# First MLP of a fused attention and MLP kernel: first eight units taken one by one, powers in another order

## The reference

```python
q_pool = q.reshape(B, H, S // 2, 2, D).mean(axis=3)
attn = softmax(q_pool @ k^T / sqrt(D));  x = attn @ v        # 2 x 8 heads
# first MLP, d_ff 2048
h = x @ w_in;  h2 = h * h;  h3 = h2 * h
P = a[0] + a[1] * h + a[2] * h2 + a[3] * h3
Q = 1.0 + np.abs(b[0]) * np.abs(h) + np.abs(b[1]) * h2
x = (P / (Q + 1e-06)) @ w_out
# second MLP, d_ff 1536
rms = sqrt(mean(x * x) + 1e-06);  xn = x / rms * rms_g
out = (silu(xn @ w_gate) * (xn @ w_val)) @ w_out2
```

## Time and profile before

| | us |
|---|---|
| median of 3 runs | 706.7 (705.28 to 706.94) |
| the profiled execution | 705.85 |
| its span, first to last instruction | 704.1 |
| TensorE busy | 687.2 (98%) |
| VectorE busy | 528.6 (75%) |
| ScalarE busy | 419.8 (60%) |
| GpSimd busy | 412.6 (59%) |

### The profile page before, as it was taken

The page is one execution under the profiler, slowest core; times in us unless marked ns, Lnnn a source line. Parts: engine busy times, 40 slices in busy tenths (PEclk is TensorE's granted clock), DMA queues, the critical chain, the costliest instruction groups (busy, mean ns, idle before and its releaser), DMA issues.

```text
span 704.1 us, 11967 instructions
## 1 busy us (share of the span) xinstructions
PE 687.2 (98%) x4068; PEld 641.4 (91%) x4068; DVE 528.6 (75%) x1033; ACT 419.8 (60%) x867; POOL 412.6 (59%) x386
## 2 busy tenths in 40 slices
PE   8799999999999997999999999999999999999998
PEld 5799999999999997899999999989999999999996
DVE  6699999999899987988988898987554444444442
ACT  5577878778777769987888877964521111111110
POOL 5766695967869756978888798866444421000000
PEclk9999999999999999999999999999999999999999
DMA  7332322224220021011101101111310300000012
GB/s 270 127 106 78 140 86 88 94 84 141 91 86 17 2 65 55 24 38 61 61 1 61 60 3 59 60 61 61 119 61 1 116 5 0 1 1 1 0 46 90
DMA packets 18027, 44.35 MB, mean 63 GB/s; under 512 B 1984, under 2 KB 2880, under 8 KB 17856
## 3 DMA queue, kind: packets, MB, share of 16 engines
q1 hardware_dynamic: 17696, 43.39, 18.2%
q10 hardware_dynamic: 288, 0.39, 0.2%
HBM read 41.42 MB, written 2.36 MB: 62 GB/s over the span
## 4 chain that ended last, share of the span: by engine, by line
PE 89%; ACT 4%; DVE 3%; DMA 2%; issue 1%; SPq 1%; POOL 0%; ACTq 0%; POOLq 0%
PE hb L618 33%; PE ob L659 23%; PE sc L508 11%; PE sc L516 9%; PE pv_ps L534 6%; PE misc L534 5%; DMA krawA<-in_k 2%; DVE neg_part L894 1%; ACT den L788 1%; ACT num L790 1%; ACT lin L791 1%; DVE pt_lo L905 0%; PE xb L612 0%; ACT hb L807 0%; PE pv_ps L553 0%
## 5 line engine op out<-in xcount | busy, mean ns | idle before, releaser
L729 ACT ACTIVATE pt_hi<-sc 128x384 fp32r<-128x384 f32 x216 | 90.5, 492 | 54.0 <-PE sc L516 54.0
L894 DVE TENSOR_REDUCE neg_part<-sc 128x1 f32<-128x384 f32 x216 | 108.3, 551 | 14.5 <-PE sc L508 12.6
L618 PE MATMUL hb<-xt_hi,wi_hi 128*128 128x384 f32 x336 | 113.9, 339 | 4.1 <-DVE gt_lo L997 3.8
L618 PE MATMUL hb<-xt_lo,wi_hi 128*128 128x384 f32 x336 | 113.1, 337 | 0.0
L618 PE MATMUL hb<-xt_hi,wi_lo 128*128 128x384 f32 x336 | 112.7, 336 | 0.0
L905 DVE TENSOR_TENSOR pt_lo<-sc,pt_hi 128x384 fp32r<-128x384 f32 x216 | 106.6, 548 | 6.1 <-ACT pt_hi L729 5.3
L659 PE MATMUL ob<-wo_hi,gt_hi 128*128 128x512 f32 x252 | 98.6, 391 | 1.5 <-DVE gt_lo L997 1.5
L659 PE MATMUL ob<-wo_lo,gt_hi 128*128 128x512 f32 x252 | 99.1, 393 | 0.0
L659 PE MATMUL ob<-wo_hi,gt_lo 128*128 128x512 f32 x252 | 99.0, 393 | 0.0
L720 ACT ACTIVATE prob<-sc,neg_max 128x1152 f32<-128x1152 f32 x72 | 89.2, 1239 | 3.2 <-DVE neg_max L898 3.2
L516 PE MATMUL sc<-ident,prob 128*128 128x128 f32 x648 | 83.1, 274 | 0.6 <-ACT prob L720 0.6
(11 more groups left out here) (140 smaller groups left out, 1637.3 us busy)
## 6 DMA issues: line engine op xcount, KB each, us to landing
wraw<-in_moe_w_out SPq DMA_DIRECT2D x7, 1024.0 KB, 5.2
qrawB<-in_q SPq DMA_DIRECT2D x8, 576.0 KB, 3.8
krawB<-in_k SPq DMA_DIRECT2D x8, 576.0 KB, 4.9
wraw<-in_moe_w_in SPq DMA_DIRECT2D x4, 1024.0 KB, 5.1
qrawA<-in_q SPq DMA_DIRECT2D x7, 576.0 KB, 4.1
krawA<-in_k SPq DMA_DIRECT2D x7, 576.0 KB, 5.0
wraw<-in_moe_w_gate SPq DMA_DIRECT2D x3, 1024.0 KB, 5.0
wraw<-in_moe_w_val SPq DMA_DIRECT2D x3, 1024.0 KB, 5.0
```

The lines of the kernel that those rows point to most:

```text
L618: ins = nc.tensor.matmul(bank[:, 0:BLOCK], w[i][:, d, col], x[j][:, d, BLOCK * nb:BLOCK * nb + BLOCK], start=d == 0 and n == 0, stop=d == ...
L729: nc.scalar.activation(pt[0][:, 3 * c:3 * c + 3, PT_COL[i]:PT_COL[i] + P], src, ACT.Copy).then_inc(pt_hi, 1)
L894: nc.vector.tensor_reduce(neg_part[:, s, c:c + 1], sc[s][:, c, 0:KBANK], AX.X, ALU.max, negate=True).then_inc(part_done, 1)
```

## The change

There are three edits. (1) `powers(u)` issues num, h2, Abs, lin in place of Abs, h2, num, lin; GpSimd waits for the first two with its product and for all four with its addition; `denominator(u)` waits for three. (2) `PROMPT = 8`: in rounds 1 to 8 the hi and lo parts of g are those of unit u-1 in place of u-2 (round 9 has none), and in rounds 0 to 7 seed and activation1 are those of unit u in place of u-1 (round 8 has none). (3) The hi and lo parts of the turned tiles stand behind seed and activation1 in place of ahead of them, and tile 6 is turned at unit 4 in place of unit 3.

```diff
--- before.py
+++ after.py
@@ -60,7 +60,9 @@
 
 RAW_AT = {45: 0, 46: 1, 47: 2}
 
-TURNED_AT = {1: (4, 5), 3: (6,), 5: (7,), 6: (8,)}
+TURNED_AT = {1: (4, 5), 4: (6,), 5: (7,), 6: (8,)}
+
+PROMPT = 8
 
 GROUPS = [(0, 1, 1, 64, 256, 0), (0, 4, 0, 0, 320, 256), (1, 6, 1, 0, 320, 576), (1, 8, 0, 0, 256, 896)]
 
@@ -474,9 +476,10 @@
 
             for u in range(UNITS * NC1):
                 h2, _, nm, ln = tmp[u % 3]
-                pool.wait_ge(h_evac, 4 * u + 4)
+                pool.wait_ge(h_evac, 4 * u + 2)
                 nc.gpsimd.tensor_tensor(nm[:], nm[:], h2[:], ALU.mult).then_inc(num, 1)
                 pool.wait_ge(num, 2 * u + 1)
+                pool.wait_ge(h_evac, 4 * u + 4)
                 nc.gpsimd.tensor_tensor(nm[:], nm[:], ln[:], ALU.add).then_inc(num, 1)
 
                 for j, n in behind_units(u):
@@ -785,9 +788,9 @@
                 if u >= 3:
                     act.wait_ge(g_full, u - 2)
                 src = hb[u % 4][:, 0:BLOCK]
+                nc.scalar.activation(nm[:], src, ACT.Identity, scale=neg_a[:, 3:4], bias=neg_a[:, 2:3]).then_inc(h_evac, 1)
+                nc.scalar.activation(h2[:], src, ACT.Square).then_inc(h_evac, 1)
                 nc.scalar.activation(den[:], src, ACT.Abs, scale=abs_b[:, 0:1]).then_inc(h_evac, 1)
-                nc.scalar.activation(h2[:], src, ACT.Square).then_inc(h_evac, 1)
-                nc.scalar.activation(nm[:], src, ACT.Identity, scale=neg_a[:, 3:4], bias=neg_a[:, 2:3]).then_inc(h_evac, 1)
                 nc.scalar.activation(ln[:], src, ACT.Identity, scale=neg_a[:, 1:2]).then_inc(h_evac, 1)
 
             def g_hi_part(u):
@@ -831,12 +834,16 @@
             last = UNITS * NC1 - 1
             for u in range(UNITS * NC1):
                 powers(u)
-                if u >= 2:
+                if 1 <= u <= PROMPT:
+                    g_hi_part(u - 1)
+                elif u > PROMPT + 1:
                     g_hi_part(u - 2)
+                if u < PROMPT:
+                    seed(u)
+                elif u > PROMPT:
+                    seed(u - 1)
                 for t in TURNED_AT.get(u, ()):
                     tokens_hi(t, False)
-                if u:
-                    seed(u - 1)
                 if u in RAW_AT:
                     tokens_hi(RAW_AT[u], True)
                 for c, t in behind(u - 1, 0):
@@ -973,7 +980,7 @@
             def denominator(u):
 
                 h2, den, _, _ = tmp[u % 3]
-                dve.wait_ge(h_evac, 4 * u + 2)
+                dve.wait_ge(h_evac, 4 * u + 3)
                 nc.vector.scalar_tensor_tensor(out=den[:], in0=h2[:], scalar=abs_b[:, 1:2], in1=den[:], op0=ALU.mult, op1=ALU.add).then_inc(den_a, 1)
 
             def activation1(u):
@@ -1032,14 +1039,18 @@
             last = UNITS * NC1 - 1
             for u in range(UNITS * NC1):
                 denominator(u)
-                if u >= 2:
+                if 1 <= u <= PROMPT:
+                    g_lo_part(u - 1)
+                elif u > PROMPT + 1:
                     g_lo_part(u - 2)
                 if u in RAW_AT:
                     tokens_scale(RAW_AT[u])
+                if u < PROMPT:
+                    activation1(u)
+                elif u > PROMPT:
+                    activation1(u - 1)
                 for t in TURNED_AT.get(u, ()):
                     tokens_lo(t, False)
-                if u:
-                    activation1(u - 1)
                 if u in RAW_AT:
                     tokens_lo(RAW_AT[u], True)
                 for c, t in behind(u, 0):
```

## The result

| | before | changed |
|---|---|---|
| median | 706.75 us (4 runs, 705.28 to 706.94) | 713.8 us (4 runs, 713.52 to 714.11) |
| profiled execution, its span | 705.85, 704.1 | 713.52, 711.7 |
| mean granted clock | 0.998 | 0.993 |

The ratio is 1.0105, 95% interval 1.009 to 1.012: 7.05 us slower. The forecast was 712.1, the range 709.0 to 714.8.

What follows compares the result with a forecast made beforehand. TensorE was taken as the bound, with gains or losses only ahead of 287 us, where ScalarE sets the pace. Unit 8's product 4.9 later plus 0.5 at the stage's end gave +5.4, 712.1 us; range 709.0 to 714.8.

Steps and rivals of the forecast that it cites:

- All four waits on gt_lo: TensorE's waits at the head of the first MLP: all go, 5.3 us of idle time, 6.1 with lost overlap.
- FP(8) later by 4.9: TensorE's first product of unit 8 waits for tile 8's lo part and starts at 294.2 against 289.38.
- Unit 0: Nothing covers its ScalarE-VectorE round trip: unit 1's powers start 1.7 us later, at 267.5, between 1.0 and 2.4.
- The stall per unit: ScalarE's Ln waits for den, held by GpSimd's product: about 0.22 us per unit, 1.3 us over six.
- The clock at 0: TensorE's granted clock may fall at the 4.2 us pause, but the loss is hidden: 0, bounds 0 and 1.7 us.
- rival (c): TensorE's clock falls at the last pause as well, 1.7 us more: 713.8 us; chance 0.13.
- A clock under 1.00 after FP(8): Sign of being wrong: TensorE's granted clock below full behind unit 8's first product.
- Order of the powers: num and h2 first, Abs third: den ends 2.56 us after S, the start of the unit's first power.
- The end of the stage: The second MLP's first product waits for a tile's lo part behind den: 0.5 us more, bounds 0 and 0.6.
- (a): Shorter lag wins: tiles' lo parts don't hold TensorE, only the four waits count, 5.3 us go, 701.4; chance 0.10.
- (b): No change, 706.7 us: tile 8 late by no more than the semaphore's reserve; chance 0.07.
- (d): VectorE becomes the bound from 287 on, each den taking 1.66 us: 2.6 us more, 714.7; chance 0.08.

Runs made afterwards that it cites:

- x1: The changed kernel with the turned tiles' hi and lo parts put back ahead of seed and activation1, tile 6 still at unit 4: 709.27 us, ratio 1.006.
- x7: The changed kernel with the last three tiles each turned a unit earlier (6 at 3, 7 at 4, 8 at 5), still behind seed and activation1: 708.34 us, ratio 1.003.
- x5: The changed kernel with GpSimd's product of unit 0 alone waiting for all four powers, as before the change: 712.86 us, ratio 1.0101.
- x4: The changed kernel with 14 matmuls of no use (2.4 us) in the pause ahead of unit 8's product: 712.6 us, ratio 1.0099.
- x2: The kernel before with only the order of the powers changed (num, h2, Abs, lin, and the waits that follow): 705.63 us, ratio 0.9994.
- x6: The changed kernel with tiles ahead of seed and activation1, turned a unit earlier, and unit 0's GpSimd product behind all four powers: 706.4 us, ratio 1.0006.

## Why the prediction was right, and what it mis-sized

**The mechanism held, step by step.** All four waits on gt_lo go; waits on xt_lo at FP(4), tile 8's transposes and FP(8) come (shown by the trace, and by x1 and x7, which move nothing but the tiles). The pauses are 4.3, 2.9 and 2.9 us of idle time, to which about 0.2 of overlap each comes in the count of the forecast, 3.5, 4.2 and 3.1. The second was smaller because FP(4) to FP(6) ran later, in part at the lower clock; tile 6 came later too, the transposes went 26.3 behind FP(0) against 25.0 forecast, but by less. Tile 6's move to unit 4 alone wasn't tried; it is not what holds FP(8), for tile 8's transposes end at 287.6 and ScalarE, without idle time ahead of it, takes tile 8's hi part at 292.81.

**FP(8) later by 4.9 was too small: 6.15.** Two terms. Unit 0: I took 1.7 us between 1.0 and 2.4; counted from FP(0) it was 2.7. The order on GpSimd and VectorE was that of my upper bound (product, divide, addition, den): den(0) ended 6.13 behind FP(0) against 5.57 forecast, 0.56 of the 1.0; the rest is the 0.39 between den's end and Ln, for which my sum had nothing (its 0.03 is what passes between Ln and Exp). The stall per unit: I took 0.22; a round without a tile takes 3.75 (276.85 to 280.60) against my 3.66, since 0.10 passes between den's end and Ln (270.84 to 270.94), for which I had 0.02, and from unit 1's powers to tile 8's hi part it is 24.5 us against 24.1. My 294.2 is 33.37 behind FP(0), so the 4.9 is 4.8 in this count, and with 1.0 and 0.4 more it becomes 6.2. x5 qualifies the first: shifting GpSimd away from unit 0 moves the start and gains only 0.3 at FP(8), so unit 0's term is not a simple addend, as it was in my sum.

**The clock at 0 was wrong: 1.7.** This was rival (c). My reason was that the pause of 4.2 would bring the clock down and shorten the last one. The pause ahead of the transposes was 2.9 instead, and the clock stood at 1.00 behind it; it fell at FP(4) and again at FP(8), where no wait followed that could hide it. "A clock under 1.00 after FP(8)" was one of my own signs of being wrong, and it came. x4 shows the price, 1.5 us, by filling the pause. The Trainium skill's "TensorE: Matmul & The Clock Gate", section "HAM oscillation — how this bites in real kernels", names gaps between bursts as what re-throttles the array; the trace agrees for 4.34 and 2.89 us and not for the 2.93 us pause at 287.00.

**Order of the powers.** den ends 0.42 behind GpSimd's product, at S + 2.55 against S + 2.56 forecast. The rule of the Trainium skill's "SBUF — State Buffer" (section "SBUF: two separate sides") that the two exclude each other held for L480 too: in units 0 to 8 no den ends inside a product. Its cost alone, with the old lag, is nothing (x2): with the seed a round behind, Ln has no den to wait for.

**The end of the stage.** I took 0.5; the wait ahead of FP(48) grew from 0.27 to 0.53, and x2 has the same 0.52, so it is the order of the powers. 0.3 us.

**Rivals.** (a) falls, though half of it is true: the short lag takes most of the waits on gt_lo away, 5.3 us before, 1.3 in x1, 0.6 in x6. (b) falls. (c) came: the clock did fall at the last pause. (d) falls: den averages 0.95 us from 304 to 440, less than the 1.13 of the earlier trace rows, and TensorE doesn't wait there:

```profile
L984 DVE SCALAR_TENSOR_TENSOR den<-h,abs_b,den 128x384 f32<-128x384 f32 x33 | 31.2, 946 | 10.2 <-ACT den L793 10.2
```

The sum, measured for forecast: 6.15 for 4.9, 1.7 for 0, 0.3 for 0.5, less 0.5 outside the stage: 7.6 for 5.4 in the spans, 7.05 for 5.4 in the medians. That the median lies at rival (c)'s 713.8 to the digit is luck in part: FP(8) came 1.25 later than (c) has it, the end of the stage cost 0.2 less, and 0.5 in the spans and another 0.5 between spans and medians went the other way.

## What to carry to other kernels

A wait that isn't in the view of waits may be the next bound: look for the reader that starts 0.1 us behind its releaser, and count what the change puts ahead of that releaser on its own engine. Shortening one chain on an engine that is busy throughout lengthened another here; move the side work (here the tiles) first, then the lag. And judge changes of 1 us by distances inside one trace, from a common instruction to the next fixed one, where the runs around them differ by 3.

## What the hardware showed beyond that

- Pauses of nearly the same length differ in what they do to the clock: 2.93 us (changed kernel, transposes) left it at 1.00, 2.89 us eight us later brought it to 0.57 over 4 us; in x5 a pause of 2.77 us brought 0.50 from 288 to 292. The fall behind FP(8) cost 1.5 to 1.7 us (x4's distance and the clock's share); the deeper fall at FP(4) in x4 cost nothing, as a wait for another engine followed it.
- With GpSimd's two tensor_tensor instructions back to back, VectorE's two instructions with two SBUF operands were both held: the divide (1.12 us for 0.49) ended 0.34 behind the product, and den(0) (1.35 for 0.61), which came when the addition already ran, 0.42 behind the addition.
